# First network on tiles of 384 tokens instead of 512, with a preparation lead of five units instead of six

## What is computed

```python
S_re, S_im = (new_re + kv, new_im)            # new = normalised a times S, per position t
y[:, :, t] = einsum('bhd,bhde->bhe', q[:, :, t], S_re)
x = y as (3072, 384)
xn = x / rms(x) * rms_g
x = (silu(xn @ w_gate) * (xn @ w_val)) @ w_out     # first network, hidden width 1536
h = x @ w_in
out = (max(h, 0) + log1p(exp(-abs(h)))) @ w_out2   # second network, hidden width 2048
```

## Time and profile before

| | us |
|---|---|
| median of 3 runs (lowest, highest) | 1201.85 (1201.65, 1202.08) |
| the profiled execution, its own time | 1201.7 |
| its span (first to last instruction) | 1199.9 |

### The profile page before, as it was taken

The page is one execution under the profiler, slowest core; times in us unless marked ns, Lnnn a source line. Parts: engine busy times, 40 slices in busy tenths (PEclk is TensorE's granted clock), DMA queues, the critical chain, the costliest instruction groups (busy, mean ns, idle before and its releaser), DMA issues.

```text
span 1199.9 us, 18970 instructions
## 1 busy us (share of the span) xinstructions
PE 1078.1 (90%) x5495; PEld 915.0 (76%) x5495; DVE 725.9 (60%) x2227; ACT 665.8 (55%) x1184; POOL 295.6 (25%) x260
## 2 busy tenths in 40 slices
PE   0555569999999999999999999989999999999996
PEld 0444468888888788888888878868888888888885
DVE  7799988999999899999999411212221213122211
ACT  3344446566655655565655333456676666676663
POOL 0033331111111111111111115643333333333332
PEclk9999999999999899999999999989999999999999
DMA  1455542443343333334432303320010101010000
GB/s 57 112 147 151 142 140 81 122 120 104 87 113 87 89 87 112 107 100 136 115 88 73 100 1 94 113 97 1 1 53 1 53 1 52 0 52 0 26 1 27
DMA packets 63851, 91.22 MB, mean 76 GB/s; under 512 B 4624, under 2 KB 53648, under 8 KB 63760
## 3 DMA queue, kind: packets, MB, share of 16 engines
q1 hardware_dynamic: 63760, 90.15, 26.4%
HBM read 60.89 MB, written 29.24 MB: 75 GB/s over the span
## 4 chain that ended last, share of the span: by engine, by line
PE 32%; issue 32%; DVE 13%; POOL 10%; DMA 6%; ACT 4%; SPq 1%; DVEq 1%; POOLq 0%; ACTq 0%
PE gbank L1329 14%; POOL pl L543 10%; PE ybank L1329 8%; DVE prep L835 5%; DMA rows_scratch<-pk 3%; PE sbank L1346 3%; DMA mm<-rows_scratch 2%; PE xbank L1358 2%; PE xbank L1357 2%; DVE pk L835 2%; PE xbank L1337 1%; PE xbank L1361 1%; ACT front L562 1%; DVE ga L835 1%; DMA a_in<-in_a 1%
## 5 line engine op out<-in xcount | busy, mean ns | idle before, releaser
L1329 PE MATMUL gbank<-xh,slab 128*128 128x512 f32 x1296 | 406.0, 395 | 3.4 <-issue 2.0
L1329 PE MATMUL ybank<-ph,slab 128*128 128x512 f32 x1020 | 319.6, 395 | 4.9 <-ACT ytile L657 4.0
L1329 PEld LDWEIGHTS gbank<-xh,slab 128*128 128x128 f32 x1296 | 242.5, 190 | 52.8 <-issue 2.1
L1329 PE MATMUL gbank<-xl,slab 128*128 128x512 f32 x648 | 254.0, 392 | 0.0
L1329 PEld LDWEIGHTS ybank<-ph,slab 128*128 128x128 f32 x1020 | 189.3, 189 | 43.2 <-issue 5.7
L518 POOL TENSOR_TENSOR pl<-hid,ph 128x512 fp32r<-128x512 f32 x72 | 98.8, 1372 | 467.6 <-ACT ph L650 467.6
L1329 PE MATMUL ybank<-pl,slab 128*128 128x512 f32 x510 | 199.6, 391 | 0.0
L543 POOL TENSOR_TENSOR pl<-hid,ph 128x512 fp32r<-128x512 f32 x96 | 125.7, 1310 | 268.2 <-ACT ph L772 268.2
L1213 DVE SCALAR_TENSOR_TENSOR hid<-gbank,hid 128x512 f32<-128x512 f32 x72 | 49.7, 691 | 214.5 <-ACT hid L763 214.5
L1329 PEld LDWEIGHTS gbank<-xl,slab 128*128 128x128 f32 x648 | 122.5, 189 | 26.3
L1337 PE MATMUL xbank<-ident,mm 96*128 96x96 f32 x192 | 28.3, 277 | 95.3 <-DMA mm<-rows_scratch 74.5
(11 more groups left out here) (126 smaller groups left out, 1597.1 us busy)
## 6 DMA issues: line engine op xcount, KB each, us to landing
rows_scratch<-pk SPq DMA_DIRECT2D x24, 771.0 KB, 4.9
mm<-rows_scratch SPq DMA_DIRECT2D x96, 192.8 KB, 4.0
a_in<-in_a SPq DMA_DIRECT2D x24, 384.0 KB, 4.7
kq_in<-in_kq SPq DMA_DIRECT2D x24, 384.0 KB, 5.8
ytile<-in_w SPq DMA_DIRECT2D x36, 192.0 KB, 4.7
prep<-in_w SPq DMA_DIRECT2D x32, 192.0 KB, 2.5
y_scratch<-ytile SPq DMA_DIRECT2D x7, 768.0 KB, 5.4
v_in<-in_v SPq DMA_DIRECT2D x24, 192.0 KB, 4.5
```

What stands on the lines that cost most here:

```text
L1329: last = pe.matmul(out, slab[:, slot + part, cols], x, start=f, stop=l)
```

## The change

The first network's tile becomes 384 tokens (three units): eight tiles instead of six. Each tile still has 12 blocks, so each of its three steps has four blocks instead of three, of 384 columns instead of 512. LEAD becomes 5: the network starts after steps 0 to 4, and 19 steps have both preparation and network blocks. The weights of the first network are loaded in steps 1 to 4 instead of 2 to 5. The loop over pairs of tiles runs three times over six steps instead of twice over eight. Fourth blocks are added at the end of each engine's step; several pieces of DVE's step change places (`p_of` of the first block behind `scaled_a`, `mask(m, 0)` behind `after_sums(1)` and `x_mean`, `state_add(m, 0)` ahead of `decay_column`, `mask(m, 1)` ahead of `odd_products`, the third and fourth `p_of` at the end of the preparation, `x_low` behind `queries`). In the last tile the first split of the second network's input (`x2_split(0, 0)`, `x2_low(0, 0)`) still follows step i = 2, which now is the tile's last. The scratch tensor of the outputs becomes one row of tokens, so that tiles of 384 can be written and tiles of 512 read.

```diff
@@ -31,8 +31,10 @@
 UNITS_B = S // CH
 NU = B * UNITS_B
 TOK = 512
-UT = TOK // CH
 NT = B * S // TOK
+TOK1 = 384
+UT = TOK1 // CH
+NT1 = B * S // TOK1
 F1 = 1536 // P
 F2 = 2048 // P
 NBK, BK = CH // 8, 8
@@ -40,7 +42,8 @@
 PAD = 24
 HH = H // 2
 ROW = 2 * CH + 1
-LEAD = 6
+LEAD = 5
+FS = F1 // UT
 LAG = 1
 
 SUM_LIMIT = -2000.0
...
@@ -381,24 +384,24 @@
 
             def store_y(T):
-                sp.dma_start(y_d[T], ytile[:, :, :]).then_inc(y_stored, 16)
+                sp.dma_start(y_d[:, :, bass.ds(T * TOK1, TOK1)], ytile[:, :, 0:TOK1]).then_inc(y_stored, 16)
 
             def load_y(T):
-                after((x2_lo, 3 * T), (y_stored, 16 * (T + 3)))
-                sp.dma_start(y2_in, y_d[T + 1]).then_inc(x2_loaded, 16)
-
-            def tile(T, last=False):
+                after((x2_lo, 3 * T), (y_stored, 16 * (4 if isinstance(T, int) and T == 0 else NT1 + 2)))
+                sp.dma_start(y2_in, y_d[:, :, bass.ds(TOK1 + T * TOK, TOK)]).then_inc(x2_loaded, 16)
+
+            def tile(T, odd, last=False):
                 for i in range(UT):
-                    n, m = 4 * T + LEAD + i, 4 * T + 5 + i
+                    n, m = UT * T + LEAD + i, UT * T + LEAD - 1 + i
                     step(n if not isinstance(n, int) or n < NU else None,
-                         m if not isinstance(m, int) or m < NU else None, (LEAD + i) % 2)
+                         m if not isinstance(m, int) or m < NU else None, (UT * odd + LEAD + i) % 2)
                     if i == 1:
                         store_y(T)
-                    if last and i == 2:
+                    if last and i == 1:
                         load_y(0)
                     if last:
-                        for r in range(3):
-                            load_w2(3 * i + r)
+                        for r in range(FS):
+                            load_w2(FS * i + r)
 
             sp.dma_start(gain[:, :], g_d.broadcast_to([P, DM])).then_inc(gain_in, 16)
             load_a(0)
...
@@ -408,21 +411,19 @@
             sp.wait_ge(mask_out, 16)
             for i in range(BK):
                 sp.dma_start(causal[i * NBK:(i + 1) * NBK, :], mask_d[i::BK, :]).then_inc(mask_in, 16)
-            step(1, 0, 1)
-            with sp.Fori(0, 2) as k:
-                step(2 * k + 2, 2 * k + 1, 0, w1=6 * k)
-                step(2 * k + 3, 2 * k + 2, 1, w1=6 * k + 3)
-            with sp.Fori(0, 2) as t:
-                tile(2 * t)
-                tile(2 * t + 1)
-            tile(4)
-            tile(5, last=True)
+            for k in range(LEAD - 1):
+                step(k + 1, k, (k + 1) % 2, w1=3 * k)
+            with sp.Fori(0, NT1 // 2 - 1) as t:
+                tile(2 * t, 0)
+                tile(2 * t + 1, 1)
+            tile(NT1 - 2, 0)
+            tile(NT1 - 1, 1, last=True)
 
             def store_out(T):
...
                                    ALU.subtract).then_inc(lo_done, 1)
 
             def tile(T, last=False):
-                for i in range(UT):
-                    if last and i:
-                        w2_lo_of(3 * i - 1)
-                    lo(T, 3 * i)
-                    if last:
-                        w2_lo_of(3 * i)
-                    lo(T, 3 * i + 1)
-                    if last:
-                        w2_lo_of(3 * i + 1)
-                    lo(T, 3 * i + 2)
+                for f in range(F1):
+                    if last and f:
+                        w2_lo_of(f - 1)
+                    lo(T, f)
                 if last:
                     w2_lo_of(F1 - 1)
 
             with pool.Fori(0, F1) as f:
...
-                    act.activation(ytile[:, m, :], ybank[m][:, :], ACT.Copy).then_inc(y_act, 1)
+                    act.activation(ytile[:, m, 0:TOK1], ybank[m][:, 0:TOK1], ACT.Copy).then_inc(y_act, 1)
 
             def step(n, m, x, par=0, col=0, T=None, i=0, w1=None, last=False):
                 more = n is not None and not (isinstance(n, int) and n + 1 >= NU)
                 if n is not None:
                     mid_w2(n)
                 if T is not None:
-                    silu(T, 3 * i)
+                    silu(T, FS * i)
                 if n is not None:
                     mid_rest(n)
                 if w1 is not None:
                     w1_hi(w1)
                 if T is not None:
-                    hi(T, 3 * i)
+                    hi(T, FS * i)
                 if last and i:
-                    w2_hi_of(3 * i - 1)
-                if T is not None:
-                    silu(T, 3 * i + 1)
+                    w2_hi_of(FS * i - 1)
+                if T is not None:
+                    silu(T, FS * i + 1)
                 if T is not None and (n is not None or x is not None):
                     act.preload_act_table_set(LN_EXP)
                 if x is not None:
@@ -688,9 +683,9 @@
                     front_r0(n + 1)
                     in_time(n + 1)
                 if T is not None:
-                    hi(T, 3 * i + 1)
+                    hi(T, FS * i + 1)
                 if last:
-                    w2_hi_of(3 * i)
+                    w2_hi_of(FS * i)
                 if w1 is not None:
                     w1_hi(w1 + 1)
                 if m is not None:
@@ -698,17 +693,22 @@
                 if T is not None and i == 0:
                     y_out(T)
                 if T is not None:
-                    silu(T, 3 * i + 2)
+                    silu(T, FS * i + 2)
+                if last:
+                    w2_hi_of(FS * i + 1)
                 if w1 is not None:
                     w1_hi(w1 + 2)
                 if m is not None:
                     kt_copy(m, 1)
                 if T is not None:
-                    hi(T, 3 * i + 2)
+                    hi(T, FS * i + 2)
+                    silu(T, FS * i + 3)
                 if last:
-                    w2_hi_of(3 * i + 1)
+                    w2_hi_of(FS * i + 2)
                 if x is not None:
                     xh_of(x, par, col, T)
+                if T is not None:
+                    hi(T, FS * i + 3)
                 if m is not None:
                     y_copy(m, 1)
 
...
@@ -1082,10 +1082,10 @@
                     state_add(m - 1, 1)
                 if n is not None:
                     scale(n)
-                if T is not None:
-                    p_of(T, 3 * i)
-                if n is not None:
                     scaled_a(n)
+                if T is not None:
+                    p_of(T, FS * i)
+                if n is not None:
                     scan(n, 0)
                     pairs_re(n)
                     scan(n, 1)
@@ -1101,15 +1101,14 @@
                 if n is not None:
                     total(n)
                 if T is not None:
-                    p_of(T, 3 * i + 1)
+                    p_of(T, FS * i + 1)
                 if n is not None:
                     after_products(n, 1)
-                if m is not None:
-                    mask(m, 0)
-                if n is not None:
                     after_sums(n, 1)
                 if x is not None:
                     x_mean(x)
+                if m is not None:
+                    mask(m, 0)
                 if n is not None:
                     after_products(n, 2)
                 if n is not None and not (isinstance(n, int) and n + 1 >= NU):
@@ -1119,15 +1118,15 @@
                 if n is not None:
                     end_1(n)
                     after_sums(n, 2)
-                if x is not None:
-                    x_second(x)
-                if n is not None:
                     end_2(n)
                     after_products(n, 4)
                 if x is not None:
+                    x_second(x)
+                if n is not None:
+                    end_3(n)
+                if x is not None:
                     x_root(x)
                 if n is not None:
-                    end_3(n)
                     after_sums(n, 4)
                     end_root(n)
                 if x is not None:
@@ -1145,33 +1144,35 @@
                     decay(m, 1)
                 if n is not None:
                     scaled_frame(n)
+                if m is not None:
+                    state_add(m, 0)
+                if n is not None:
                     decay_column(n)
                     last_products(n)
                     carry_of(n)
                     last(n)
-                if m is not None:
-                    state_add(m, 0)
-                if n is not None:
                     middle_products(n)
                     query(n)
                     middle(n)
-                if T is not None:
-                    p_of(T, 3 * i + 2)
-                if n is not None:
-                    odd_products(n)
                 if m is not None:
                     mask(m, 1)
                 if n is not None:
+                    odd_products(n)
                     odd(n)
                     even_products(n)
+                if T is not None:
+                    p_of(T, FS * i + 2)
```

(85 more changed lines are left out.)

40 lines of the change are left out of this document (19 added, 21 removed).

## The result

The changed kernel takes 1214.26 us (median of 4 runs, 1212.48 to 1216.54) against 1201.75 for the kernel before (4 runs, 1200.55 to 1202.08): ratio 1.0111, with a 95% interval of 1.0099 to 1.0124. It is slower by 1.1%; the two medians are 12.5 us apart.

The account below looks back on a forecast made before the run. The prediction took a closed loop of waits through PE, ACT and DVE, 28.05 us a step against PE's own 27.05, as the bound. Its terms added +10.3 us to 1201.7, giving 1212 us, range 1194 to 1223.

Parts of the forecast that it names:

- opening: Steps ahead of the first network blocks: 149.45 us instead of 174.47, so -25.0 us, bounds -28 and -23.
- first network step: First step with network blocks: PE need not work itself so far ahead of DVE, -1.7 us (0 to -3).
- steady steps: Steps with preparation and network blocks: 19 at 28.0 us, set by the PE-ACT-DVE-PE loop, against 483.5 before: +48.5 us.
- pass starts: Loop over tiles starting anew, two instead of one, each priced at DVE's 3.4 us gap: +1.7 us (-3 to +5).
- rest of the first network: First network's end, after the steps with preparation: 104.3 us instead of 118.92, so -14.6 us.
- second network: Way into the second network: 5.5 us idle instead of 4.05, shorter output groups, late weight splits; +1.4 us.
- 384 columns: PE's wide matmuls: 173.3 ns each, taking 13.3 ns on top as fixed per matmul.
- rival 2: PE's wide matmuls: the 13.3 ns go with the columns, 170 ns each, total 1206 us; chance 0.14.
- rival 4: PE's wide matmuls: weight loads set the spacing, 190 ns say, +1.8 us on 24 steps, 1255 us; chance 0.02.
- DVE beside POOL: DVE's part of the loop: POOL's split holds DVE up, but 0.3 us less, as the split gets shorter.
- Rival 1: Wait of kt_of(m, 1) for state_add(m, 0): loop does not close, steps of 27.05, 18 us less, 1194; chance 0.24.
- Rival 3: Near-tied paths, pk back late or first-half masks late: 28.5 us a step, 1225 us in all; chance 0.12.

Follow-up runs that it names:

- a_front_first: Changed kernel with front_sq(n + 1) moved ahead of products_by_row(n) on ACT; 1202.6 us, 1.0008 of the kernel before.
- last two experiments: Kernel before and changed kernel, both with loop written out, front_sq ahead of products_by_row, a_in loaded ahead of mm; 1225.93 and 1213.24 us.
- b_both: Kernel before with front_sq ahead of products_by_row on ACT and the loop over pairs of tiles written out; 1198.49 us, 0.9947.
- b_both_a_early: Kernel before, loop written out, front_sq ahead of products_by_row, and a_in loaded ahead of load_mm(m, 0) on SP; 1225.93 us, 1.0161.

## Why the prediction was right, and what in it was not

The forecast was 1212.0 us, the median 1214.26; slower, as it was most likely to be. By its own terms, against spans (the start of PE's wide matmuls at 150.29, forecast 151, belongs to the first):

| term | forecast | measured | from |
|---|---|---|---|
| opening | -25.0 | -26.0 | stores at 148.49 and 174.47 |
| first network step | -1.7 | -3.1 | 29.78, 1.9 over a steady one; before 5.0 over |
| steady steps | +48.5 | +45.7 | 19 x 27.85 - 483.5 |
| pass starts | +1.7 | +10.2 | 8.5 + 6.9 - 5.1 (with 27.85) |
| rest of the first network | -14.6 | -15.3 | 103.65 - 118.92 |
| second network | +1.4 | -0.2 | 412.69 - 412.85 |
| sum | +10.3 | +11.3 | |

- **Steady step.** 28.05 by the four parts, 27.83 measured: PE 6.38 against 6.28, ACT 5.57 against 5.55, DVE 5.52 against 5.49, PE 10.58 against 10.51. Each part came within 0.1, and that this loop sets the step is shown by two edits that moved it both ways. PE's wait was 0.58 instead of about 1, since 27.83 is less and a smaller wait of 0.23 stands before `outputs(m, 0)`.
- **Opening.** The first step with weights took 32.41, forecast 31.9; the three behind it 29.5, 29.2 and 29.2, together 1.3 us less than at the 29.75 taken.
- **384 columns.** 173.3 ns, as taken; rival 2 (170.0, 3.06 us for 18) and rival 4 (3.4) are out. The Trainium skill (TensorE: Matmul & The Clock Gate, section Back-to-back issue gap) states its N/2.4 + 2.5 ns for an isolated matmul, which the prediction left out; for a sustained stream of matmuls with weight loads it gives some 131 ns at 512 columns. These trains agree with the form of the formula, 13.3 ns over N/2.4 at either width. They agree neither with its 2.5 ns nor with the 131 (226.7 here).
- **DVE beside POOL.** The hold is still in DVE's part of the loop, and as short as forecast: POOL's split and, beside it, the `frame` sums on DVE.

```profile
573.21 1.04 POOL L519 TENSOR_TENSOR pl<-hid,ph 128x384 fp32r<-128x384 f32 x1 [9.01 <-ACT ph L645]
```

```profile
573.41 0.94 DVE L835 TENSOR_TENSOR frame<-cu,cw 128x3 f32<-128x3 f32 x2
```

  Two sums of three columns took 0.94 us and ended within 0.1 us of the split's end. The Trainium skill (SBUF — State Buffer, section SBUF: two separate sides) says that a VectorE operation with two SBUF inputs and a GpSimd operation exclude one another for the whole instruction; this row goes with it, as did. No run took the POOL operation away.
- **Pass starts: the term that was mis-sized.** The step was "I price each at DVE's gap, 3.4". Measured were 8.5 and 6.9. DVE's gap itself was 4.99 and 4.94, not the 3.38 of the earlier trace rows; and I had counted neither that PE, which now runs behind DVE, waits 3.49 and 2.87 more for DVE's mask, nor the low clock behind that wait. I had argued from the wide matmuls that stand ahead of PE's gap. Behind that gap of 1.33 us the clock did stay at 1.00; behind the 3.49 us it was at 0.50, though nine wide matmuls stand ahead of that wait too. The row of before had the warning in it: 5.1 over, at a clock of 0.90. Pricing each start at that whole 5.1 would have given +5.1, half of what came. Why DVE's gap is longer after the change stays open.
- **Why the total still fit.** The steady steps (2.8 less), the opening and the first step (2.4 less together), the rest (0.7 less) and the transition (1.6 less) made up for 8.5 too little on the pass starts. The forecast was nearer than its terms, and that part is luck.
- **Rival 1** named the right place: with the loop shortened by ACT's exchange, steps went to 27.03. The changed kernel itself did not do that. Its price of 18 us was too high; a_front_first won 11.7 by the medians.
- **Rival 3** (ties give way, 28.5 a step): not in the changed kernel, where PE ran 1.87 us behind DVE (557.78 against the store at 555.91; 1.6 forecast) without a wait for `mm`. The last two experiments show how near it was: with the load of `mm` issued behind that of the input, and its median landing 0.6 to 0.8 us later (4.2 to 4.8, 3.9 to 4.7), it binds in nearly every step.
- **Into the second network.** PE's gap was 4.71 instead of 5.5: DVE's three splits took 2.70, not the 4.34 of the earlier trace rows that the forecast had taken over. Which part of the 1.6 us in this term that came out below the forecast is due to that, and which to the +1 for weights split late, is not shown.

## What to carry to other kernels

When a bigger or smaller tile moves a kernel's balance, write the step as a closed loop through the engines, part by part, and compare its length with the bound engine's own work; the difference is what an exchange of two neighbours can win, down to the next path and no further, so look up the second and third wait before you price it. Price a jump back of a long loop by the whole excess of the step in which it happens, low clock included, and not by one engine's gap; here each cost 5 to 9 us, and writing the loop out gave it back. A saving at the start and the end of a pipeline (26 and 15 us here) can pay for steady steps that are a little longer, but only after those taxes are gone.

## What the runs showed of the hardware that was not expected

- At the start of a pass of a long loop three engines stood without anything to wait for: DVE 4.99 us, ACT 2.95, PE 1.33 in the step from 317.60 on, and PE's granted clock over the step was 0.86. With the loop written out none of this was there.
- One change in the order of the loads that SP issues, with the same bytes, moved the median landing of `mm` from 3.9 to 4.7 us, and the time against the kernel before from 0.9947 to 1.0161 (b_both and b_both_a_early).
- The same 18 matmuls of 384 columns took 3.12 us at a granted clock of 2.4 GHz and 5.36 us with most of them at 1.2 GHz, behind a wait of 3.49 us; behind a gap of 1.33 us the clock had stayed at 2.4 GHz.
